# A fused attention, FFN and slot-mixture kernel: the stretch behind the last FFN unit is rebuilt

## The reference

```python
# attention over 32 (batch, head) pairs: 576 pooled queries, 1152 keys, head size 64 -> x, 2304 tokens x 512
h = x @ w_in                                    # 512 -> 2048
g = np.where(h > 0.0, h, np.exp(np.minimum(h, 0.0)) - 1.0)
y = g @ w_out                                   # 2048 -> 512
# slot mixture: 8 experts x 4 slots = 32 slots, hidden size 1024
logits = y @ phi                                # 2304 x 32
d = exp(logits - logits.max(0)); d /= d.sum(0) + 1e-09      # over tokens
slot_input = d.T @ y                            # 32 x 512
slot_out[e] = relu(slot_input[e] @ w1[e]) @ w2[e]           # 4 slots of each expert
c = exp(logits - logits.max(1)); c /= c.sum(1) + 1e-09      # over slots
return c @ slot_out                             # 2304 x 512
```

## Time and profile before

| what | value |
|---|---|
| time, median of 3 runs | 959.31 us (959.04 to 960.89) |
| the profiled execution's own time | 959.24 us |
| its span | 957.5 us |
| PE busy | 919.3 us, 96% |
| DVE / ACT / POOL busy | 520.9 / 395.7 / 362.8 us |
| DMA traffic | 76.32 MB |

### The profile page before, as it was taken

One profiled execution on the slowest core, in us unless ns is written; L12 is line 12 of the kernel. 1 busy time (PEld: TensorE's weight loads), 2 busy tenths in 40 slices (PEclk: granted clock), 3 DMA queues, 4 the chain that ended last, 5 costly groups with the idle time before them and its releaser, 6 DMA issues.

```text
span 957.5 us, 16643 instructions
## 1 busy us (share of the span) xinstructions
PE 919.3 (96%) x6450; PEld 701.9 (73%) x6450; DVE 520.9 (54%) x919; ACT 395.7 (41%) x734; POOL 362.8 (38%) x263
## 2 busy tenths in 40 slices
PE   5899999999999999999999999999999999999794
PEld 3566656666666666655899999999999999999342
DVE  5867766676667666756564433433433433433333
ACT  3555555565555555647342222232232232232102
POOL 1878888888888888888000000000000000000000
PEclk9999999999999999999999999999999999999898
DMA  6112112222122022303320000200000000456795
GB/s 233 46 55 76 62 39 75 76 76 75 51 75 75 29 73 75 92 1 111 102 75 1 1 1 1 88 1 1 1 1 1 1 1 1 170 215 255 298 381 198
DMA packets 36126, 76.32 MB, mean 80 GB/s; under 512 B 2896, under 2 KB 11216, under 8 KB 36048
## 3 DMA queue, kind: packets, MB, share of 16 engines
q1 hardware_dynamic: 36048, 75.26, 22.1%
HBM read 70.53 MB, written 4.72 MB: 79 GB/s over the span
## 4 chain that ended last, share of the span: by engine, by line
PE 50%; POOL 2%; DVE 1%; ACT 1%; DMA 0%; issue 0%; POOLq 0%; ACTq 0%; DVEq 0%
PE psum L645 7%; PE psum L627 7%; PE psum L629 7%; PE psum L646 7%; PE psum L647 7%; PE psum L628 7%; POOL acc L1315 2%; PE psum L722 2%; PE psum L757 1%; PE psum L678 1%; PE psum L684 1%; PE psum L660 0%; PE psum L576 0%; DMA out<-ob 0%; PE psum L665 0%; PE psum L745 0%
## 5 line engine op out<-in xcount | busy, mean ns | idle before, releaser
L1315 POOL TENSOR_TENSOR acc<-acc,pt 128x576 f32<-128x576 f32 x220 | 312.9, 1422 | 58.2 <-ACT pt L856 30.0
L856 ACT ACTIVATE pt<-psum 128x576 f32<-128x576 f32 x288 | 183.1, 651 | 130.4 <-PE psum L563 130.1
L562 PE MATMUL psum<-qs,kraw 64*128 64x288 f32 x576 | 184.0, 405 | 0.0
L563 PE MATMUL psum<-qs,kraw 64*128 64x288 f32 x576 | 183.9, 405 | 0.0
L1034 DVE TENSOR_REDUCE mx<-psum 128x1 f32<-128x512 f32 x256 | 162.1, 676 | 17.9 <-PE psum L507 16.2
L576 PE MATMUL psum<-pt,vs 128*64 128x288 f32 x1152 | 153.6, 411 | 0.0
L1207 DVE TENSOR_SCALAR gf<-gf 128x384 f32<-128x384 f32 x96 | 34.5, 360 | 195.7 <-ACT gf L976 195.7
L645 PE MATMUL psum<-gh,W 128*128 128x384 f32 x384 | 133.4, 347 | 0.0
L976 ACT ACTIVATE gf<-psum 128x384 f32<-128x384 f32 x96 | 47.2, 492 | 200.8 <-PE psum L629 200.2
L646 PE MATMUL psum<-gl,W 128*128 128x384 f32 x384 | 128.5, 335 | 0.0
L629 PE MATMUL psum<-xh,W 128*128 128x384 f32 x384 | 128.4, 334 | 0.0
(11 more groups left out here) (137 smaller groups left out, 1323.0 us busy)
## 6 DMA issues: line engine op xcount, KB each, us to landing
ring<-in_w SPq DMA_DIRECT2D x32, 1024.0 KB, 7.2
qraw<-in_qT SPq DMA_DIRECT2D x16, 576.0 KB, 4.8
kraw<-in_kT SPq DMA_DIRECT2D x16, 576.0 KB, 3.6
vs<-in_v SPq DMA_DIRECT2D x16, 576.0 KB, 3.8
out<-ob SPq DMA_DIRECT2D x9, 512.0 KB, 6.6
wst<-in_w_in SPq DMA_DIRECT2D x16, 256.0 KB, 2.7
wst<-in_w_out SPq DMA_DIRECT2D x16, 256.0 KB, 2.9
sel<-in_selection SPq DMA_DIRECT2D x1, 96.0 KB, 8.9
```

The costliest lines, as they stand in the source:

```text
L562: mm(lo, kraw[0:64, p % NB, keys], qs[0:64, p % NB, q], start=False, stop=True).then_inc(s_Ta, 1)
L563: mm(hi, kraw[64:P, p % NB, keys], qs[64:P, p % NB, q], start=False, stop=True).then_inc(s_Tb, 1)
L856: act.activation(pt[:, i % NPT, :, :], t_pair(("T", h, kt))[:, :, 0:HALF], ACT.Exp, scale=SCALE)\
L1315: pool.tensor_tensor(a, first, pt[:, i % NPT, :, :], ALU.add).then_inc(s_acc, 1)
```

## The change

Only the part behind the last `stage2` is rewritten, and one memset of a PSUM bank is put at DVE's start (the memsets of the tail are gone; TensorE's first score product waits for it). The last chunk's y is read bank by bank, ACT taking banks 0 and 2, DVE 1 and 3, each as soon as its own matmuls are through (`s_yl`). Its logits are read from PSUM by the maximum and by the exponential; the copy `lts` is made later, by ACT. The YTR results go to the banks of y, and ACT copies two, DVE one. S comes in two halves of 256 columns; the totals are inverted while it runs; the slot inputs are made by matmuls of `s_run` with `add_inv`, a matrix that adds the three copies and scales by the inverse. CT is a plain transpose of three tiles at once, in two groups (chunks 0 to 3, then 4 and 5), with no split, and stands ahead of DTR and behind `layer1(0)`. `layer1(1)` waits for the second group's copy (`s_ct`). The layers' parts are put in another order. SO comes in halves. The 18 products are plain fp32 over 32 rows, the rows going round over three row groups, and each gives its own signal. Places in SBUF change for `cT`, `sinT`, `so` and `hidT1`, which no longer lie under the ring.

```diff
+        def last_rows(j):
+            if j == 2:
+                pe.wait_ge(s_ytok, 3 * LAST + 1)
+            for t in range(PB):
+                ins = nc.tensor.transpose(last_rows_bank(j)[:, t * P:(t + 1) * P], yT[:, t, j * TT:(j + 1) * TT],
+                                          ident[:, :])
+            ins.then_inc(s_yr, 1)
+
+        def token_weights(group):
+            for n, i in enumerate(CT_GROUPS[group]):
+                pe.wait_ge(s_c, i + 1)
+                ins = nc.tensor.transpose(ct_bank(group)[0:3 * NS, n * TT:(n + 1) * TT], c_all[:, 3 * i:3 * i + 3, :],
+                                          ident[:, :])
+            ins.then_inc(s_CT, 1)
+
+        def last_slot_sums(k):
+            item = ("S", LAST, k)
+            h_wait(item)
+            cols = slice(k * DM // 2, (k + 1) * DM // 2)
+            for j in range(3):
+                ins = mm(h_bank(item)[NS * j:NS * j + NS, 0:DM // 2], d_tok[:, j, :], y[:, j, cols], start=True, stop=True)
+            ins.then_inc(s_H, 1)
...
+            pe.wait_ge(s_srun, 2 * LAST + 1 + k)
+            for t in range(2):
+                at = (2 * k + t) * P
+                ins = mm(h_bank(item)[:, t * NS:(t + 1) * NS], s_run[:, at:at + P], add_inv[:, :], start=True, stop=True)
+            ins.then_inc(s_H, 1)
+
+        slot_item(("LP", LAST))
+        last_rows(0)
+        slot_item(("LT", LAST))
+        last_rows(1)
+        last_rows(2)
+        token_weights(0)
+        slot_item(("DTR", LAST))
+        pe.wait_ge(s_dtok, LAST + 1)
+        pe.wait_ge(s_y1, 1)
+        pe.wait_ge(s_ytok, 3 * LAST + 2)
+        for k in range(2):
+            last_slot_sums(k)
         pe.wait_ge(s_fin, 4)
-        pe.wait_ge(s_z, 2)
...
+        for k in range(2):
+            slot_inputs(k)
+        pe.wait_ge(s_lts, 1)
+        slot_item(("LTR", LAST))
+
+
+        def layer1(gr, part):
+            if gr == 0 and part % 2 == 0:
+                pe.wait_ge(s_sin, part // 2 + 1)
+            if gr:
+                pe.wait_ge(s_ct, 2)
+            at, landed, _ = slot(number(gr, 0, part))
...
-        layer1(0)
+        def slot_outputs(gr):
+            pe.wait_ge(s_sow, gr + 1)
...
+        for part in range(4):
+            layer1(0, part)
+        token_weights(1)
+        layer1(1, 0)
         hidden_transposed(0)
-        layer1(1)
-        for part in range(4):
+        for part in range(1, 4):
+            layer1(1, part)
+        layer2(0, 0)
+        hidden_transposed(1)
+        for part in range(1, 4):
             layer2(0, part)
-        hidden_transposed(1)
-        for i in range(NCT):
-            token_weights(i)
-            if i == NCT - 1 or i % 2:
-                layer2(1, i // 2)
+        layer2(1, 0)
+        layer2(1, 1)
+        slot_outputs(0)
+        layer2(1, 2)
         layer2(1, 3)
-
...
-        pe.wait_ge(s_ct, NCT)
+        slot_outputs(1)
+
+
+
         pe.wait_ge(s_so, 1)
-        for r in range(NROUND):
-            if r >= 4:
-                pe.wait_ge(s_fa, r - 3)
-                pe.wait_ge(s_fd, r - 3)
-            for k in range(2):
-                i = 2 * r + k
-                ins = mm(psum[:, i % 8, :], cT[:, i * P:(i + 1) * P], so[:, :], start=True, stop=True)
-            ins.then_inc(s_fo, 1)
+        pe.wait_ge(s_sod, 1)
+        for i in range(NT // P):
+            if i >= 8:
+                pe.wait_ge((s_fa, s_fd)[i % 2], (i - 8) // 2 + 1)
+            rows = slice(NS * (i % 3), NS * (i % 3) + NS)
+            mm(psum[:, i % 8, :], cT[rows, i // 3, :], so[rows, :], start=True, stop=True).then_inc(s_fo, 1)
...
-            act.copy(yT[:, 0:2, :], psum[:, Y_BANKS[0]:Y_BANKS[1] + 1, 0:CH]).then_inc(s_ya, 1)
+            if c < LAST:
+                act.copy(yT[:, 0:2, :], psum[:, Y_BANKS[0]:Y_BANKS[1] + 1, 0:CH]).then_inc(s_ya, 1)
+            else:
+                act.copy(yT[:, 0, :], psum[:, Y_BANKS[0], 0:CH]).then_inc(s_ya, 1)
+                act.wait_ge(s_yl, 3)
+                act.copy(yT[:, 2, :], psum[:, Y_BANKS[2], 0:CH]).then_inc(s_ya, 1)
...
-        read_parts(NCH - 1)
-        read_rows(NCH - 1, 0)
-        slot_exp(NCH - 1)
-        read_rows(NCH - 1, 1)
-        read_rows(NCH - 1, 2)
-        token_exp(NCH - 1)
-        for i in range(NCT):
-            item = ("CT", i)
-            act.wait_ge(s_H, h_at[item] + 1)
-            act.wait_ge(s_x1, 4 * piece(CT_PIECE)[0] + piece(CT_PIECE)[2] + 1)
-            act.copy(cT[:, i * CH:(i + 1) * CH], h_bank(item)[0:3 * NS, 0:CH]).then_inc(s_cth, 1)
...
+        read_parts(LAST)
+        last_read_rows(0)
+        slot_exp(LAST)
+        last_read_rows(2)
+        last_logits()
+        read_token_weights(0)
+        token_exp(LAST)
+        read_token_weights(1)
         act.wait_ge(s_H, h_at[("SO", 0)] + 1)
-        act.copy(so[:, :], h_bank(("SO", 0))[0:3 * NS, :]).then_inc(s_soh, 1)
+        act.copy(so[:, 0:DM // 2], h_bank(("SO", 0))[0:3 * NS, 0:DM // 2]).then_inc(s_so, 1)
...
-        c = NCH - 1
-        slot_max(c)
-        dve.wait_ge(s_ya, NCH)
-        dve.wait_ge(s_yd, NCH)
-        weights_by_token(c)
-        dve.memset(psum[:, Y_BANKS[0]:Y_BANKS[1] + 1, :], 0.0).then_inc(s_z, 1)
-        running_sum(c)
-
-        tot, inv = slot_st[:, 8:9], slot_st[:, 9:10]
...
-        dve.wait_ge(s_fin, 2)
-        dve.tensor_scalar(s_run[:, :], s_run[:, :], inv, None, ALU.mult).then_inc(s_fin, 1)
-        dve.memset(psum[:, Y_BANKS[2]:Y_BANKS[3] + 1, :], 0.0).then_inc(s_z, 1)
-        dve.wait_ge(s_H, h_at[("SIN", 0)] + 1)
-
...
+        last_slot_max()
+        last_read_rows()
+        weights_by_token(LAST)
+        inverse_totals()
+        for k in range(2):
+            last_running_sum(k)
+        for k in range(2):
+            read_slot_inputs(k)
+        token_max(LAST)
+        token_norm(LAST)
+        for gr in range(2):
+            hidden_relu(gr)
+            read_hidden(gr)
+        outputs_wide(0)
         outputs_wide(1)
-        dve.wait_ge(s_soh, 1)
-        part = so[NS:2 * NS, :]
-        dve.tensor_tensor(part, h_bank(("SO", 0))[NS:2 * NS, :], part.bitcast(F32), ALU.subtract).then_inc(s_so, 1)
+        dve.wait_ge(s_H, h_at[("SO", 1)] + 1)
+        dve.tensor_copy(so[:, DM // 2:DM], h_bank(("SO", 1))[0:3 * NS, 0:DM // 2]).then_inc(s_sod, 1)
```

More of the change, by code:

```diff
@@ L344, in h_bank, with last_rows_bank, ct_bank @@
         return psum[:, H_BANKS[h_at[item] % 4], :]
+    def last_rows_bank(j):
+        return psum[:, Y_BANKS[j % 2], :]
+    CT_GROUPS = (range(0, 4), range(4, NCT))
+    def ct_bank(group):
+        return psum[:, Y_BANKS[2 + group], :]
     def piece(n):
@@ L696, in _ @@
                     stage2(c, f - 2)
[L697 to L708, removed]
@@ L711, in _ @@
-        pe.wait_ge(s_fin, 4)
-        pe.wait_ge(s_z, 2)
-        def layer1(gr):
-            for part in range(4):
[L715 to L725, removed]
+        def last_rows(j):
[5 more added lines that the diff above has]
+            ins.then_inc(s_yr, 1)
@@ new lines, in _ @@
+        slot_item(("DTR", LAST))
[4 more added lines that the diff above has]
+            last_slot_sums(k)
+        pe.wait_ge(s_fin, 4)
+        for k in range(2):
[8 more added lines that the diff above has]
+            at, landed, _ = slot(number(gr, 0, part))
+            for half in landed:
+                pe.wait_ge(*half)
+            wp = at.rearrange("p (e n) -> p e n", e=4)
+            for half in range(2):
+                for j in range(4):
+                    e = 4 * gr + j
+                    ins = mm(psum[32 * j:32 * j + SE, Y_BANKS[2 * gr + half], :],
+                             sinT[:, part, SE * e:SE * e + SE],
+                             wp[:, j, half * 512:(half + 1) * 512], start=(part == 0), stop=(part == 3))
+            ins.then_inc(s_x1, 1)
@@ L944, in slot_exp @@
         def slot_exp(c):
-            act.wait_ge(s_lt, 3 * c + 3)
+            act.wait_ge(s_lt, 3 * c + 2 if c == LAST else 3 * c + 3)
             if c:
                 act.wait_ge(s_H, h_at[("DTR", c - 1)] + 1)
+            logits = h_bank(("LT", c))[0:3 * NS, 0:CH] if c == LAST else lts[:, :]
             new = slot_st[:, c % 2:c % 2 + 1]
@@ L951, in slot_exp @@
                 act.wait_ge(s_srun, 2 * (c - 1))
-            act.activation(dT[0:3 * NS, :], lts[:, :], ACT.Exp, bias=new,
+            act.activation(dT[0:3 * NS, :], logits, ACT.Exp, bias=new,
                            accum_out=slot_st[:, 2 + c % 2:3 + c % 2]).then_inc(s_d, 1)
@@ L1254, in _, with last_slot_max @@
-        token_max(c)
-        token_norm(c)
-        def outputs_wide(gr):
-            dve.wait_ge(s_x2, 4 * gr + 4)
-            dve.tensor_copy(so_wide[:, gr, :], psum[:, Y_BANKS[2 * gr], :]).then_inc(s_sow, 1)
-        for gr in range(2):
+        def last_slot_max():
+            lt = h_bank(("LT", LAST))[0:3 * NS, 0:CH]
+            new, old, cur = (slot_st[:, k:k + 1] for k in (LAST % 2, 1 - LAST % 2, 6))
+            dve.wait_ge(s_H, h_at[("LT", LAST)] + 1)
+            dve.wait_ge(s_d, LAST)
```

(5 more changed lines are left out.)

153 lines of the change are left out of this document (95 added, 58 removed).

## The result

The changed kernel takes 948.13 us (median of 4 runs, 948.07 to 948.27), the kernel before 959.28 beside it (4 runs, 959.04 to 960.89): a ratio of 0.988, 95% interval 0.9863 to 0.9898. The profiled execution takes 948.27, with a span of 946.5.

A forecast was written before the change was run, and what follows sets the result against it. Bound by a chain of waits: FFN matmuls, engine-to-engine steps, TensorE's experts, then output DMA. Experts ending at 928.8 plus 19.6 behind them gave a 948.4 span, 9.1 less, so 950.2 us; range 948.8 to 953.8.

The forecast's parts named there:

- The experts' start: From the last FFN matmuls to the experts' first matmul: start at 897.2 in place of 901.00, 3.8 us earlier.
- S, given at 894.7: S, ahead of the slot inputs, can begin at 894.67 in place of 896.30, a gain of 1.63 us.
- The experts: First to last expert matmul: 31.6 us in place of 36.40, ending at 928.8.
- the gap for ACT's copy: Ahead of layer1(1): a new wait of 1.0 us for two transposes and ACT's copy of the second group.
- transfers and TensorE nearly tie: At the experts' end: weight transfers give 928.7, TensorE's matmuls 928.8, so a faster front brings nothing more.
- Behind the experts: From the last expert matmul to the span's end: 19.6 us in place of 20.10, from copy, products and output.
- the second and third rivals: Output products: without overlap on three row groups, 952.5 us (chance 0.08); so slow that the kernel loses time (0.02).
- The last 15.19 stay: Output stage, first output issue to the span's end, DMA writing 4.72 MB: kept at 15.19 us.
- the tail 0.4 shorter: Behind the experts: part of the range's lower bound of 948.8, with the landing bounding the experts a microsecond earlier.
- The first rival, the clock: TensorE's clock falls again behind the FFN, slowing the experts' first products by 1.5 to 3.4 us: 951.7 to 953.6, chance 0.31.
- Slower: Whole kernel slower than before, through output products needing 1.34 us each against 0.29 forecast; chance 0.02.
- no change: Gains lost to unseen waits: the chain would have to stand 7 us longer somewhere; chance 0.03.

The follow-up runs named there:

- the last unedited profile: The changed kernel, unedited, run beside the three with work added to the tail: median 950.52 us, ratio 0.9901 to the kernel before.
- the run with transposes: The changed kernel with 16 transposes added (ten behind the transposes of dT, six behind S) into an unread bank: 949.93 us, ratio 0.9894.
- 5 + 3 products: The changed kernel with eight small matmuls added (five behind the transposes of dT, three behind S) into an unread bank: 949.27 us, ratio 0.9885.

## Why the prediction was right and wrong

**The experts' start**, 3.8 earlier by forecast, came 4.0 earlier counted from the FFN's end. S, given at 894.7, stood at 893.30; 1.06 of that is the FFN's end, 0.3 the rest. The copies of the first three banks cost nothing, as forecast. The last one, 887.94 to 888.50, stands inside LP: up to LP's end (889.39 in place of 890.94) 0.46 is gained, where 0.42 was forecast.

**The experts**: the pattern held, the size was 0.92 too small. Without a wait for DMA (the last unedited profile, where they take 32.26 from 895.88 on), the seven runs of expert matmuls take 28.34, where I had 27.5 and 0.2 for one end. By these rows every switch to transposes and back costs an end of about 0.1 to 0.2 (an estimate: 64 matmuls take 6.98 ahead of a switch and took 6.87 in the run of before that I used), not only the last one. SO's half took 1.03 for 0.9; the gap for ACT's copy was 0.81 for 1.0. In the recorded profile the DMA wait adds 0.29. That transfers and TensorE nearly tie was right: TensorE's waits for the last piece are 0.3 us in the result's profile, 0.3 to 0.7 in four others, 1.6 in the run with transposes, and none in four (96 and 192 instructions more, 5 + 3 products, the last unedited one); a fall of the clock does not decide which.

**Behind the experts** 4.42 came for 4.45, and the products overlap on three row groups, so the second and third rivals (products one by one) are out.

**The failed step is "The last 15.19 stay".** I took the output stage of one profile as a property of 4.72 MB. It is 13.6 for the writes and 1.6 for an instruction packet that happened to fall into them. The change makes the programs shorter (16478 instructions of all engines in the trace in place of 16643) and with it moves the packets; so of the 11.15 gained by medians 1.6, as the profiles have it, come from where the packet fell and not from a faster tail, and 96 instructions that do nothing bring the kernel before down by 2.1 by medians. The rows to see it by were in the trace of before: nine issues that end at 951.5, the bulk at 954.8, and one engine writing alone for 1.7 us. Second, I kept the FFN's end fixed, where it moves by over a microsecond with the clock's first rise; that is a matter of the range, whose lower bound of 948.8 had no room for either. The range's low end was reckoned from the transfers and "the tail 0.4 shorter" alone.

**The first rival, the clock**, had 0.31 and was put at 951.7 to 953.6. It is real: 949.8 to 951.5 us in the executions of the unedited kernel with a fall (5 of 12), none in the 4 of the result. Its price, forecast as 1.5 to 3.4, is 1.2 to 1.7 in the three profiles that have it; by their times the executions with a fall lie 1.5 to 3.6 above those without (947.9 to 948.3), and the two longest were not profiled. So the result's time owes something to luck: four more executions of the same kernel, three with a fall, have a median of 950.52, near the forecast, but there a cost that the forecast's sum had left out makes up for the two that it had too high. All four profiles of the kernel before and its two variants have a fall, of 6.8 to 10.2 us; the change shortens it to 3.4 or avoids it. "Slower" and "no change" are excluded by every run.

## What to carry to other kernels

A stage that a change does not touch is not a constant: before a profile's duration is carried over, ask what in it is there by chance (a code packet among the output's writes, one DMA engine still busy behind the others, when the clock first rose), and give the range room for it. Compare two traces stage by stage, each from its own start, or a shift from far ahead passes for a gain. Where transfers and TensorE tie, take the time off the one that ends last, and look at several executions before a fall of the clock, or its absence, is put down to the change.

## What the runs showed of the hardware

- A code packet of 16 KB among the output's writes made the output 0.85 to 1.6 us longer, with a last stretch at a sixteenth of the DMA rate; instructions that do nothing, far ahead, move it in or out.
- The clock's first rise came between 20.4 and 23.6 us in the profiles here, under the same work but for one memset, and the FFN's end 866 us later followed it (887.8 to 889.1).
- Whether the clock falls behind the FFN (from 1.00 to 0.50 of 2.4 GHz) differed between executions of the changed kernel: 13 of 28 without work added to its tail, none of 12 with it. In the seven profiles without, it went with the moment of the first rise; why is open.
